# VectorE's routing inside both branches of attention, and eight more unread matmuls on TensorE

## The reference

```
# attention
scores = q @ k.T / 8 + bias(head, distance)      # kept: the first n_global keys and the n_local before each query
out    = softmax(scores where kept) @ v          # to x: (1536, 512)
# first expert layer: one of 8 experts for each token, or none
compute = x @ w_skip > 0
e_idx   = argmax(x @ w_gate);  gate = softmax(x @ w_gate)[e_idx]
x       = x + gate * (relu(x @ w1[e_idx]) @ w2[e_idx])   where compute
# second expert layer: 4 experts, all for each token
out     = sum over e of p[:, e] * (relu(x @ w1[e]) @ w2[e]),  p = domain_probs / sum
```

## Time and profile before

| | us |
|---|---|
| median of 3 runs | 757.61 |
| lowest, highest | 757.59, 758.4 |
| the profiled execution | 757.19 |
| its span, first to last instruction | 755.3 |
| around the span | 1.89 |

### The profile page before, as it was taken

How to read it: one execution, slowest core, us unless ns; L and a number is a source line. 1 busy time by engine, 2 the same in 40 slices (tenths; PEclk the granted TensorE clock), 3 DMA queues, 4 the chain that set the end, 5 groups by cost and what they waited for, 6 DMA issues and landing times.

```text
span 755.3 us, 11207 instructions
## 1 busy us (share of the span) xinstructions
PE 734.7 (97%) x4155; PEld 648.9 (86%) x4156; DVE 465.2 (62%) x932; ACT 324.7 (43%) x585; POOL 78.1 (10%) x114
## 2 busy tenths in 40 slices
PE   8999998799999899999999999999999999999996
PEld 4899898587888789899898898998989989899895
DVE  5776766798989976743753653564474275265442
ACT  3665665498988634322341330422333134043130
POOL 3101000126337000000000000000000000000203
PEclk8999999799999999999999999999999999999998
DMA  9869950799977210110110030030011002000102
GB/s 156 170 150 286 252 178 26 262 387 375 331 270 109 85 42 1 59 53 1 41 72 1 1 112 1 1 111 0 0 56 56 0 2 109 0 0 0 56 28 83
DMA packets 85969, 74.11 MB, mean 98 GB/s; under 512 B 52642, under 2 KB 58788, under 8 KB 85924
## 3 DMA queue, kind: packets, MB, share of 16 engines
q1 hardware_dynamic: 81924, 64.97, 28.5%
q0 software_dynamic: 3456, 8.43, 4.3%
q10 hardware_dynamic: 544, 0.13, 0.1%
HBM read 67.19 MB, written 6.33 MB: 97 GB/s over the span
## 4 chain that ended last, share of the span: by engine, by line
PE 92%; DVE 4%; issue 1%; ACT 1%; DMA 0%; SPq 0%; POOLq 0%; POOL 0%; DVEq 0%
PE ps L2176 34%; PE ps L2155 29%; PE ps L2053 12%; PE ps L1862 3%; PE ps L1887 2%; PE ps L1886 2%; PE ps L1871 2%; PE ps L1836 2%; PE ps L1905 1%; PE ps L2028 1%; PE ps L1895 1%; DVE X L1285 1%; DVE ql L1242 1%; DMA X<-in_k 0%; PE ps L2022 0%
## 5 line engine op out<-in xcount | busy, mean ns | idle before, releaser
L2155 PE MATMUL ps<-xs,w1s 128*128 128x384 f32 x1344 | 237.7, 335 | 2.5 <-DVE shared L1714 1.3
L2155 PEld LDWEIGHTS ps<-xs,w1s 128*128 128x128 f32 x1344 | 233.4, 188 | 5.6 <-DVE shared L1714 1.6
L2176 PE MATMUL ps<-w2s,h_hi 128*128 128x512 f32 x768 | 237.1, 390 | 0.0
L2176 PEld LDWEIGHTS ps<-w2s,h_hi 128*128 128x128 f32 x768 | 143.7, 188 | 29.3
L2176 PE MATMUL ps<-w2s,h_lo 128*128 128x512 f32 x384 | 149.8, 390 | 0.0
L1745 DVE SCALAR_TENSOR_TENSOR X<-ps,prn,X 128x512 f32<-128x512 f32 x84 | 63.1, 751 | 121.7 <-PE ps L2176 121.3
L1105 ACT ACTIVATE shared<-ps 128x384 f32<-128x384 f32 x94 | 45.2, 488 | 182.1 <-PE ps L2155 182.0
L1714 DVE TENSOR_TENSOR shared<-ps,shared 128x384 f32<-128x384 f32 x96 | 52.2, 556 | 91.2 <-ACT shared L1105 68.1
L2176 PEld LDWEIGHTS ps<-w2s,h_lo 128*128 128x128 f32 x384 | 72.1, 188 | 15.0
L1108 ACT ACTIVATE h_hi<-shared 128x384 fp32r<-128x384 f32 x96 | 49.7, 525 | 38.5 <-DVE shared L1714 38.5
L892 POOL DMA_INDIRECT out<-X,dst_i x12 | 11.6, 966 | 492.6 <-DVE X L1745 492.6
(11 more groups left out here) (194 smaller groups left out, 831.1 us busy)
## 6 DMA issues: line engine op xcount, KB each, us to landing
ring<-in_moe_w SPq DMA_DIRECT2D x24, 1024.0 KB, 13.1
raw<-in_moe_w SPq DMA_DIRECT2D x16, 1024.0 KB, 5.1
shared<-in_moe_w SPq DMA_DIRECT2D x8, 1024.0 KB
X<-in_v SPq DMA_DIRECT2D x16, 192.0 KB, 2.9
ys_d<-X SPq DMA_DIRECT2D x8, 384.0 KB, 3.3
X<-in_k SPq DMA_DIRECT2D x14, 192.0 KB, 4.2
shared<-in_q SPq DMA_DIRECT2D x14, 192.0 KB, 4.2
X<-in_v SPq DMA_DIRECT2D x16, 96.0 KB, 2.8
```

The lines of the kernel that those rows point to most:

```text
L2155: mm = pe.matmul(out_, w1s[:, wp, WI[name], c, f * P:(f + 1) * P], xs[:, 3 * b:3 * b + 3, xp, XI[name], c, :], start=(not onto and x == 0 ...
L2176: mm = pe.matmul(ps[:, 6 + k % 2, :], h_, w2s[:, wp, c, :], start=(x == 0 and c == 0), stop=(x == 2 and c == 3))
```

## The change

On DVE the routing up to the token list becomes a function `routing()`, which is called at the end of the taken branch and at the end of the general one; before, it stood once behind both. In it the reduction over the experts comes first, and the memset that raises `x_ready` and the memset of oh_b's last row follow it; before, these stood ahead of it, and DVE waited for its own `x_ready`. What comes behind the token list (the gates and all further) is still behind both branches. On PE the first fillers are 10 and not 9; two are new between the first transposes and the load of the flag; three are new ahead of the last transposes of attention outputs and two behind them.

```diff
--- before.py
+++ after.py
@@ -1313,6 +1313,46 @@
                 else:
                     queries_low(m, int(g[1]))
 
+            def over(a, n, axis):
+                return a.unsqueeze(axis).broadcast_to([P, n, a.shape[1]] if axis == 1 else [P, a.shape[1], n])
+
+            def note(ins):
+
+                chained[0] += 1
+                ins.then_inc(dch, 1)
+
+            before_routing = chained[0]
+
+            def routing():
+
+
+                chained[0] = before_routing
+                dve.wait_ge(const_p, 28)
+                dve.wait_ge(ld_small, 48)
+                link(dve.tensor_reduce(mx, lg[:, :, 0:E], AX.X, ALU.max))
+                dve.memset(nn[:, 12:13], 0.0).then_inc(x_ready, 1)
+                note(dve.memset(oh_b[:, NT, :], 0.0))
+                dve.tensor_tensor(dl, lg[:, :, 0:E], over(mx, E, 2), ALU.subtract).then_inc(dl_done, 1)
+                dve.wait_ge(dl_done, 1)
+                link(dve.scalar_tensor_tensor(wv, dl, 0.0, over(rev, NT, 1), ALU.is_equal, ALU.mult))
+                link(dve.tensor_reduce(v1, wv, AX.X, ALU.max))
+                link(dve.scalar_tensor_tensor(v2, lg[:, :, E], 0.0, v1, ALU.is_gt, ALU.mult))
+                dve.tensor_tensor(oh_b[:, 0:NT, :], over(rev, NT, 1), over(v2, E, 2), ALU.is_equal).then_inc(oh_done, 1)
+                dve.wait_ge(oh_done, 1)
+                note(dve.tensor_scalar(oh_p[:, 0:NT, :], oh_b[:, 0:NT, :], pidx1, None, ALU.mult))
+                note(dve.tensor_tensor(oh_t[:, 0:NT, :], oh_b[:, 0:NT, :], over(tile0, E, 2), ALU.mult))
+
+
+                dve.wait_ge(rk_done, 1)
+                link(dve.tensor_tensor(tmp8, oh_b[:, 0:NT, :], ps[:, 3, 0:NT * E].rearrange("p (t e) -> p t e", e=E), ALU.mult))
+                link(dve.tensor_reduce(rank, tmp8, AX.X, ALU.add))
+                for t in range(NT):
+                    dve.tensor_scalar(onehot[:, t, :], iota_rb, rank[:, t:t + 1], None, ALU.is_equal).then_inc(one_done, 1)
+                note(dve.tensor_copy(tally, ps[:, 3, NT * E:(NT + 1) * E]))
+                link(dve.tensor_scalar(least.rearrange("p t e -> p (t e)"), ps[:, 3, 0:NT * E], float(P), None, ALU.min))
+                dve.wait_ge(tb_done, 1)
+                dve.tensor_copy(tok_i[:, 0:E], ps[:, 4, 0:E]).then_inc(tok_done, 1)
+
             with dve.If(f > 0):
                 keys_low(0, 0)
                 queries_low(0, 0)
@@ -1349,6 +1389,7 @@
                 normalise(NB - 1, 1)
                 add_logits(NB - 1)
                 dve.wait_ge(lg_add, NB)
+                routing()
             with dve.Else():
                 dve.wait_ge(const_p, 24)
                 dve.wait_ge(k_hi, 1)
@@ -1421,42 +1462,7 @@
                     dve.wait_ge(x_st[b], 16 * HP)
                 for x in range(2):
                     unit_low(0, x)
-            dve.memset(nn[:, 12:13], 0.0).then_inc(x_ready, 1)
-
-            dve.wait_ge(x_ready, 1)
-            dve.wait_ge(const_p, 28)
-            dve.wait_ge(ld_small, 48)
-
-            def over(a, n, axis):
-                return a.unsqueeze(axis).broadcast_to([P, n, a.shape[1]] if axis == 1 else [P, a.shape[1], n])
-
-            def note(ins):
-
-                chained[0] += 1
-                ins.then_inc(dch, 1)
-
-            note(dve.memset(oh_b[:, NT, :], 0.0))
-            link(dve.tensor_reduce(mx, lg[:, :, 0:E], AX.X, ALU.max))
-            dve.tensor_tensor(dl, lg[:, :, 0:E], over(mx, E, 2), ALU.subtract).then_inc(dl_done, 1)
-            dve.wait_ge(dl_done, 1)
-            link(dve.scalar_tensor_tensor(wv, dl, 0.0, over(rev, NT, 1), ALU.is_equal, ALU.mult))
-            link(dve.tensor_reduce(v1, wv, AX.X, ALU.max))
-            link(dve.scalar_tensor_tensor(v2, lg[:, :, E], 0.0, v1, ALU.is_gt, ALU.mult))
-            dve.tensor_tensor(oh_b[:, 0:NT, :], over(rev, NT, 1), over(v2, E, 2), ALU.is_equal).then_inc(oh_done, 1)
-            dve.wait_ge(oh_done, 1)
-            note(dve.tensor_scalar(oh_p[:, 0:NT, :], oh_b[:, 0:NT, :], pidx1, None, ALU.mult))
-            note(dve.tensor_tensor(oh_t[:, 0:NT, :], oh_b[:, 0:NT, :], over(tile0, E, 2), ALU.mult))
-
-
-            dve.wait_ge(rk_done, 1)
-            link(dve.tensor_tensor(tmp8, oh_b[:, 0:NT, :], ps[:, 3, 0:NT * E].rearrange("p (t e) -> p t e", e=E), ALU.mult))
-            link(dve.tensor_reduce(rank, tmp8, AX.X, ALU.add))
-            for t in range(NT):
-                dve.tensor_scalar(onehot[:, t, :], iota_rb, rank[:, t:t + 1], None, ALU.is_equal).then_inc(one_done, 1)
-            note(dve.tensor_copy(tally, ps[:, 3, NT * E:(NT + 1) * E]))
-            link(dve.tensor_scalar(least.rearrange("p t e -> p (t e)"), ps[:, 3, 0:NT * E], float(P), None, ALU.min))
-            dve.wait_ge(tb_done, 1)
-            dve.tensor_copy(tok_i[:, 0:E], ps[:, 4, 0:E]).then_inc(tok_done, 1)
+                routing()
 
 
             dve.wait_ge(ee_done, 1)
@@ -1818,7 +1824,7 @@
                               ones_b[:, :].unsqueeze(1).broadcast_to([P, 4, P]), start=True, stop=True)
 
             pe.wait_ge(const_p, 1)
-            unread(9)
+            unread(10)
             pe.wait_ge(const_p, 4)
 
             def bank_free(j):
@@ -1907,6 +1913,7 @@
 
             fill(0, "k0")
             fill(0, "q0")
+            unread(2)
             f = banded(pe)
             with pe.If(f > 0):
                 fill(0, "k1")
@@ -1932,7 +1939,9 @@
                 pv(NU_ - 2)
                 logits(NB - 1, 0)
                 pv(NU_ - 1)
+                unread(3)
                 outputs_T(NB - 1, 1)
+                unread(2)
                 logits(NB - 1, 1)
             with pe.Else():
                 pe.wait_ge(ld_small, 48)
```

## The result

| | before | changed |
|---|---|---|
| median of 17 runs each, us | 757.91 | 758.59 |
| lowest to highest | 756.15 to 759.57 | 757.91 to 759.49 |
| ratio | | 1.0016, 95% interval 1.0008 to 1.0023 |
| the profiled execution, its span | 757.19, 755.3 | 758.14, 756.4 |

The median lies within the range and the sign is wrong.

A forecast was written before the change was run, and what follows sets the result against it. It took PE's half clock at the start and the joint, and the joint's chain of waits, as the bound. Sum: 0 (DVE) − 0.2 (ranks) + 0 (start) from 757.61 gives 757.4 us, range 755.8 to 759.0.

The forecast's parts named there:

- the sign: Whole kernel: slightly faster, −0.2 us from the median 757.61.
- the part on the last outputs: Five fillers before the joint: fit PE's waits, clock holds over the ranks, −0.2 us (bounds 0 to 0.40), then falls.
- rival C: Joint: wider hole before gate matmuls, clock returns late, first expert's matmuls at half speed; +1.7 us, 759.1; chance 0.12.
- The jump ahead of the routing: DVE after the logits' add: reduction 0.7 us earlier, two memsets cost 0.08, so token list 0.63 us earlier.
- The jump behind the token list: DVE ahead of the gates: the jump moves here, costing 0.63 us again, so the gate chain gets 0, give or take 0.05.
- Rival D: DVE's moved jump, over 123 instructions instead of 94, waits for an instruction fetch: +2.1 us, 759.5; chance 0.07.
- The gather: Joint: issued earlier after the token list, no longer binding with 0.6 us to spare; PE's fillers are then late.
- the earlier loads: Pieces 8 and 9, loaded about 0.3 us sooner, share DMA engines with the gather but buy nothing.
- Fillers at the first loads: PE at the start: three fillers fit the waits, cost 0 (bounds 0 to 0.5), and clock gain taken as nothing.
- Rival A: Start: the clock also holds, scores of tile 2 1.16 us sooner; 756.4, or 756.1 or less with ranks; chance 0.30.
- Rival B: Start and joint: neither clock holds, only the DVE part acts; 757.6 us; chance 0.14.

The follow-up runs named there:

- run 1: Only DVE's part of the change, fillers as before, against the kernel before: 759.30 us, ratio 1.0027.
- run 7: The changed kernel with seven fillers for five ahead of the gate matmuls and five for three behind them: 756.32 us, ratio to before 0.9987.
- run 5: The kernel before with DVE's part, seven fillers for five ahead of the gate matmuls and five for three behind: 757.84 us, ratio 1.0003.
- run 2: Only the change's eight new fillers, DVE's stream as before, against the kernel before: 758.19 us, ratio 1.0013.
- run 3: Only the three new fillers at the first loads, against the kernel before: 757.09 us, ratio 1.0007.
- run 6: The changed kernel with the loads of pieces 8 and 9 only after the first gather has landed: 757.92 us, ratio to before 1.0010.
- run 9: Run 8 with pieces 8 and 9 loaded after the first gather and one filler, not six, behind the gates: 755.18 us, ratio to before 0.9977.
- run 4: Only the five new fillers at the last attention outputs, against the kernel before: 759.93 us, ratio 1.0024.
- run 8: The changed kernel with all of PE's waits in the joint (attention to first expert layer) filled by fillers: 756.45 us, ratio to before 0.9987.
- run 11: Run 8 with DVE's stream as before the change: 756.43 us, ratio to before 0.9983.
- run 12: Run 9 with DVE's stream as before the change: 756.51 us, ratio to before 0.9988.
- run 10: Run 8 without the three new fillers at the first loads: 756.95 us, ratio to before 0.9990.

## Why the prediction was wrong

The forecast's step that failed is in the part on the last outputs: "I expect the clock to fall then, some 3 us later than now, and the table and the fillers to run at half clock as before". It took the moment of the clock's return as given and counted only its fall. The clock did hold over the ranks, which gave 0.26 us where 0.2 was forecast; it fell as they ended, at 134.5, which is 0.9 us later than before and not 3. It came back at 148.1, not 143.8. The term that was missing is the first expert's block, 18 matmuls at 6.16 us and not 4.33: +1.83, and +0.53 for the transposes ahead of it. This was rival C, priced at 1.7, and its mechanism (DVE's gates stay, the fillers go, the hole grows, the return fails) is what the profiles of the changed kernel and of runs 1 and 7 show; run 5's times go with it. It had a chance of 0.12. It is not the whole account of the medians: run 2, without DVE's part, loses about as much by its ratio, and run 3's profile has the late return without a wider hole.

That the median lies in the range is luck. The start won about 1.1 us that the sum put at 0, the jumps 0.3 that it put at 0, and the late return took 2.4 that it did not have.

**The jump ahead of the routing.** Right and a little better: the reduction starts 0.03 us after the add, not 0.8, and the two memsets ran beside the subtraction, so 0.77 and not 0.63 was won.

**The jump behind the token list.** Right that it comes back, too dear: 0.47 us, not 0.63. DVE's part on the chain to the gates is −0.30, not 0. Rival D, a dearer jump, did not come.

**The gather.** The forecast called it no longer a bound, with 0.6 us to spare, and the earlier loads harmless. Both wrong: it was issued 0.7 us closer behind the loads, landed 4.4 us after its issue and bound the joint by 0.35 us. Runs 6 and 9, in which the loads wait, show 3.4 and 3.5.

**Fillers at the last outputs.** They fit their holes, as worked out. Beside the 0.26 us of the ranks they change which executions get an early return; alone they are slower (run 4).

**Fillers at the first loads.** Cost nothing, as said. Rival A came in the profiled execution: 1.02 to 1.09 us at the scores of tile 2, against 1.16 worked out. But run 1's profile, without them, also has full clock there, so this profile alone does not show that they did it. All profiles together bear it out: the four transposes at 7.4 us take 0.65 us in all nine with these fillers (changed, runs 2, 3, 6 to 9, 11, 12) and 1.11 us in four of the five without (before, runs 4, 5, 10; not run 1). Measured with the joint held they bring about 0.5 us (run 10).

**Rival B** (neither clock holds, 757.6) is nowhere. A and C came together, which the list of rivals, one case at a time, did not allow for; and the forecast went by one profiled execution where the kernel before has executions from 756.0 to 759.6.

What stays open: what decides in a given execution when the clock changes, what the slower executions of run 2 and run 4 lose and where, and why runs 9 and 12 keep some bad executions.

## What to carry to other kernels

When fillers hold TensorE's clock, any edit on another engine that moves a wait must be followed to the fillers around it, and ahead of dense work the clock's return matters more than its fall: here it cost 1.8 us at a place that the edit does not touch. A kernel whose runs spread over 3 us with the mean granted clock is judged by many runs and by the spread, and filling the joint completely gave times near before's best in every run of two kernels (a spread of 0.7 us in run 8, 0.8 in run 11). It is no guarantee: runs 9, 10 and 12, filled too, spread over 1.8 to 2.8 us. When a small gather is moved ahead, move the bulk loads behind it.

## What the runs showed of the hardware

- TensorE's clock returned to full after stretches in which it was busy 3.09 of 3.4, 2.99 of 3.3 and 3.30 of 3.3 us, and not after 2.57 and 2.17 of 3.3 (changed) or 2.67 of 3.4 and 1.99 of 3.3 (run 1). Busy time alone does not tell: it did not return after 2.98 of 3.5 in run 3 (above), nor after 3.05 of 3.4 in run 6 and 3.16 of 3.4 in run 7:

```profile
136.50:139.90 3.40, 3.05 (x18) 1.36 (x19) 2.58 (x16) 2.26 (x3) 1.39 (x2) 0.50 0.03 7
```

```profile
135.50:138.90 3.40, 3.16 (x27) 2.01 (x29) 2.72 (x17) 3.30 (x4) 0.90 (x1) 0.50 1.00 374
```

- How long the half clock lasts differs between executions of one kernel: run 4 has mean granted clocks of 0.995 and of 0.982 (756.1 and 761.2 us). In the one profile of each kernel, half clock in the joint lasted 6.8 us in runs 2, 4 and 7, 10.2 before, 13.7 changed, 17.1 in run 1 and 20.5 in run 3.
- A gather of 256 KB, issued 5.3 to 5.6 us behind the start of 2 MB of loads, landed after 4.4 to 5.0 us (changed, runs 1, 8 and 10); issued 5.8 to 6.0 us behind them, after 3.5 to 4.1 (before, runs 2, 3, 4 and 11); with the loads held back, after 3.4 to 3.5 (runs 6, 9 and 12).
- A jump of VectorE over 94 instructions cost 0.63 us behind a wait (before), one over 123 instructions 0.47 us behind a short cast (changed).
- Two small memsets behind a reduction ran beside the next instruction and cost nothing on the chain: the subtraction starts 0.30 us after the reduction, and 0.29 before.
